# A fused retention, expert and MLP kernel: the MLP reads its tokens in the order in which the experts store them

## The reference

```python
# 1. retention: 4 batches x 8 heads x 768 steps, head dimension 64
state = gamma * state + outer(k[t], v[t]);  y[t] = (q[t] @ state) / 8
# 2. mixture of experts, one expert of 8 for each token (x: 3072 x 512)
e_idx  = argmax(x @ w_gate);  probs = softmax(x @ w_gate)
eom    = sigmoid(x @ w_output_gate)
out[t] = probs[t, e] * eom[t, e] * (relu(x[t] @ w1[e]) @ w2[e])   # 512 -> 1024 -> 512
# 3. gated MLP on all tokens
xn  = x / sqrt(mean(x * x) + 1e-6) * rms_g
g   = xn @ w_gate2;  out = (g * sigmoid(g) * (xn @ w_val)) @ w_out   # 512 -> 1536 -> 512
```

## Time and profile before

| | |
|---|---|
| the profiled execution's own time | 1163.04 us |
| its span, first to last instruction | 1161.2 us |
| mean granted TensorE clock | 0.989 |
| PE busy | 1119.0 us, 96% of the span |
| PEld busy | 936.0 us, 81% |
| DVE busy | 432.2 us, 37% |
| ACT busy | 384.2 us, 33% |
| POOL busy | 135.2 us, 12% |

### The profile page before, as it was taken

How to read it: one execution, slowest core, us unless ns; L and a number is a source line. 1 busy time by engine, 2 the same in 40 slices (tenths; PEclk the granted TensorE clock), 3 DMA queues, 4 the chain that set the end, 5 groups by cost and what they waited for, 6 DMA issues and landing times.

```text
span 1161.2 us, 19477 instructions
## 1 busy us (share of the span) xinstructions
PE 1119.0 (96%) x6051; PEld 936.0 (81%) x6052; DVE 432.2 (37%) x812; ACT 384.2 (33%) x632; POOL 135.2 (12%) x188
## 2 busy tenths in 40 slices
PE   6999998999999999994999999999999999999997
PEld 5999986888888888883888888888888888888886
DVE  3777753423415415312443323322332332233222
ACT  2554432534435435423324213212231322222112
POOL 2444423201001101101100100000010010000000
PEclk9999999999999999997999999999999999999999
DMA  9989814435333533532200200020020001000001
GB/s 195 250 238 243 218 56 154 142 95 178 108 108 121 186 108 118 190 94 70 79 31 1 74 1 1 2 71 0 0 72 0 0 19 53 0 0 37 1 1 37
DMA packets 111244, 97.22 MB, mean 84 GB/s; under 512 B 79968, under 2 KB 85344, under 8 KB 111200
## 3 DMA queue, kind: packets, MB, share of 16 engines
q1 hardware_dynamic: 98624, 67.12, 20.3%
q0 software_dynamic: 6528, 21.50, 6.0%
q10 hardware_dynamic: 6048, 8.01, 2.1%
HBM read 76.43 MB, written 20.19 MB: 83 GB/s over the span
## 4 chain that ended last, share of the span: by engine, by line
PE 51%; issue 2%; ACT 1%; DMA 1%; DVE 1%; POOL 0%; POOLq 0%; SPq 0%; ACTq 0%
PE bank L630 17%; PE bank L631 17%; PE bank L632 17%; PE bank L622 0%; DVE hl L1206 0%; ACT hh L884 0%; DMA yr<-expert_rows,cur_idx 0%; DMA out_rows<-x_out 0%; POOL yr L1349 0%; ACT x_out L891 0%; ACT junk L859 0%; DVE xl L1189 0%; ACT xh L869 0%; DVE yr L1184 0%; ACT small L862 0%
## 5 line engine op out<-in xcount | busy, mean ns | idle before, releaser
L1197 DVE TENSOR_TENSOR gated<-bank,sig 128x512 f32<-128x512 f32 x72 | 49.8, 691 | 311.7 <-ACT sig L877 311.7
L630 PE MATMUL bank<-xh,w1h 128*128 128x512 f32 x384 | 149.4, 389 | 0.0
L632 PE MATMUL bank<-xh,w1l 128*128 128x512 f32 x384 | 149.4, 389 | 0.0
L631 PE MATMUL bank<-xl,w1h 128*128 128x512 f32 x384 | 149.4, 389 | 0.0
L877 ACT ACTIVATE sig<-bank 128x512 f32<-128x512 f32 x72 | 43.1, 598 | 273.2 <-PE bank L632 273.0
L630 PE MATMUL bank<-w2h,hh 128*128 128x512 f32 x288 | 113.2, 393 | 4.4 <-DVE hl L1206 4.4
L631 PE MATMUL bank<-w2l,hh 128*128 128x512 f32 x288 | 112.1, 389 | 0.0
L632 PE MATMUL bank<-w2h,hl 128*128 128x512 f32 x288 | 112.1, 389 | 0.0
L1042 DVE TENSOR_TENSOR hidl<-bank,hidh 128x512 fp32r<-128x512 f32 x58 | 39.7, 685 | 162.0 <-ACT hidh L769 162.0
L884 ACT ACTIVATE hh<-prod 128x512 fp32r<-128x512 f32 x72 | 45.5, 632 | 153.5 <-PE bank L632 133.0
L1206 DVE TENSOR_TENSOR hl<-prod,hh 128x512 fp32r<-128x512 f32 x72 | 49.9, 693 | 95.0 <-ACT hh L884 95.0
(11 more groups left out here) (185 smaller groups left out, 1881.3 us busy)
## 6 DMA issues: line engine op xcount, KB each, us to landing
stage<-in_moe_w SPq DMA_DIRECT2D x64, 512.0 KB, 5.3
expert_rows<-tile_o ACTq DMA_DIRECT2D x29, 256.0 KB, 2.3
q_raw<-in_q SPq DMA_DIRECT2D x24, 256.0 KB, 5.6
k_raw<-in_k SPq DMA_DIRECT2D x24, 256.0 KB, 6.3
v_raw<-in_v SPq DMA_DIRECT2D x24, 256.0 KB, 3.8
out_rows<-x_out SPq DMA_DIRECT2D x24, 256.0 KB, 2.8
stage<-in_moe_w_out SPq DMA_DIRECT2D x6, 512.0 KB, 3.3
stage<-in_moe_w_gate SPq DMA_DIRECT2D x5, 512.0 KB, 6.7
```

What stands on the lines that cost most here:

```text
L630: pe.matmul(out_ap, lh, rh, start=first, stop=False)
L631: pe.matmul(out_ap, lh, rl, start=False, stop=False)
L632: return pe.matmul(out_ap, ll, rh, start=False, stop=last)
L1197: v3.tensor_tensor(gated[:], bank[GV[f % 2][0]][:, :], sig[:], ALU.mult).then_inc(s["gated_done"], 1)
```

## The change

1. **Layout.** `y_dram` has 3200 rows in all. Each tile is stored right behind the rows of the experts ahead of it, so that row i of y_dram is the i-th token in expert order. The tail of a tile that an expert doesn't fill is overwritten by the next store. The routing gets some ten instructions more for `row_at`, between `index_ready` and `control_ready`.
2. **Row data.** For every token its factor and its number are stored as two words at its place in expert order (`row_meta`), by 24 indexed stores of POOL, three behind each of eight row fetches. They are read back by one DMA of 3072 pieces of 8 bytes. `gates_of_rows` gets three instructions more for the places.
3. **Loads of a block.** Blocks 1 to 5 come by one plain DMA of 1 MB each from SP in place of four gathers of POOL.
4. **Block 0** is loaded ahead of the fetch for tile 19, into the buffers `x_out` and `more_rows`; its statistics and scaling stand ahead of tile 22, half of its transposes behind tile 22, the rest behind tile 23, in PSUM banks 6 and 7. Tiles 22 and 23 are written out behind the loop.
5. **Stores.** The MLP's rows leave by indexed stores of POOL, from four buffers in place of two.
6. **Beginning.** The zero rows are written from ACT's queue behind the constants; the constants are reordered and come in four DMAs.
7. **fetch_rows(3)** stands ahead of the wait for `gates_ready`.

```diff
+XG_AT = 54 * 1024
+ROWS_FROM = SURE - 5
+FINAL_AFTER = 13
...
-        y_dram = nc.dram_tensor("expert_rows", (EXPERTS * CAP, D), U32).ap()
+        y_dram = nc.dram_tensor("expert_rows", (TOKENS + P, D), U32).ap()
+        meta_dram = nc.dram_tensor("row_meta", (TOKENS, 2), U32).ap()
...
+        def turned_bank(n, kd):
+            return bank[6 + kd % 2] if isinstance(n, int) and n == 0 else bank[GV[kd // 2][kd % 2]]
... SP
-            for e in range(2):
-                sp.dma_start(x_dram[ds(e * CAP, 1), :], no_row).then_inc(s["bases_set"], 16)
...
-            def store_block(n):
-                for t in range(BLK):
-                    sp.wait_ge(s["sum_out"], BLK * n + t + 1)
-                    sp.dma_start(out[ds((n * BLK + t) * P, P), :], x_rows[:, t % 2, :]).then_inc(out_stored[t % 2], 16)
+            def load_rows(n):
+                sp.wait_ge(s["xn_turned"], KD * n)
+                sp.dma_start(yr[:].bitcast(U32), y_dram[ds(n * BLK * P, BLK * P), :].rearrange("(t p) d -> p t d", p=P))\
+                  .then_inc(s["yrows_in"], 16)
+            sp.wait_ge(s["tile_stored"], 16 * TILES)
+            with sp.Fori(1, NBLK) as n:
+                load_rows(n)
... PE
-            with pe.Fori(LEAD, SURE) as a:
+            with pe.Fori(LEAD, SURE - 2) as a:
                 expert_tile(a)
+            expert_tile(SURE - 2)
+            turn_xn(0, [0])
+            expert_tile(SURE - 1)
+            pe.wait_ge(s["xl_ready"], 2)
+            turn_xn(0, [1])
...
-                if f == 0 and not (isinstance(n, int) and n == 0):
+                if f == 0 and isinstance(n, int) and n == 0:
+                    pe.wait_ge(s["tile_stored"], 16 * TILES)
+                elif f == 0:
                     pe.wait_ge(s["sum_out"], BLK * n)
...
-            turn_xn(0, [0, 1])
             ffn_block(0)
... ACT
+            with act.Fori(LEAD, SURE - 2) as a:
                 expert_tile(a)
+            act.wait_ge(s["early_done"], 2)
+            norm_stats(0)
+            expert_tile(SURE - 2)
+            turned_hi(0, 0)
+            turned_hi(0, 1)
+            expert_tile(SURE - 1)
+            turned_hi(0, 2)
+            turned_hi(0, 3)
...
-                    if t >= 2 or not (isinstance(n, int) and n == 0):
-                        act.wait_ge(out_stored[t % 2], 16 * ((BLK // 2) * n + t // 2))
-                    nc.scalar.activation(x_rows[:, t % 2, :], bank[SUM[t]][:, :], ACT.Copy).then_inc(s["sum_out"], 1)
+                    if not (isinstance(n, int) and n == 0):
+                        act.wait_ge(out_stored[t], 16 * n)
+                    nc.scalar.activation(out_rows(t), bank[SUM[t]][:, :], ACT.Copy).then_inc(s["sum_out"], 1)
... DVE, between index_ready and control_ready
-            also(v3.tensor_copy(row_at[:, LEAD:], src_f[0:1, LEAD:]))
+            settle(v3.tensor_tensor_scan(upto_n[:], scan_ones[:], n_e[:], 0.0, ALU.mult, ALU.add))
+            settle(v3.tensor_tensor(ahead_e[:], upto_n[:], n_e[:], ALU.subtract))
+            also(...back_e...); also(memset); also(memset)
+            settle(v3.scalar_tensor_tensor(out=skip_e[:, 1:], ...), 4)
+            settle(v3.tensor_tensor(by_skip[:], begun[0:1, :, :], ..., ALU.mult))
+            settle(v3.tensor_reduce(skip_f[:], by_skip[:], X, ALU.max))
+            settle(v3.tensor_tensor(at_f[:], con[0:1, C_ROW:C_ROW + TILES + 1], skip_f[:], ALU.subtract))
+            settle(v3.tensor_scalar(row_at[:, LEAD:], at_f[:, LEAD:], lead_n[0:1, 0:1], None, ALU.add))
...
+            dve.wait_ge(s["meta_in"], 16)
+            settle(v3.tensor_copy(row_scale[:], meta_back[:, :, 0]))
+            stage_scale(0)
+            normalise(0)
+            expert_tile(SURE - 2)
+            turned_lo(0, 0)
+            turned_lo(0, 1)
+            expert_tile(SURE - 1)
+            turned_lo(0, 2)
+            turned_lo(0, 3)
... POOL
             pool.wait_ge(s["control_ready"], 1)
+            fetch_rows(LEAD + 1)
             pool.wait_ge(s["gates_ready"], 1)
             load_early(0)
-            fetch_rows(LEAD + 1)
+            fetch_rows(LEAD + 2)
...
+            for i in range(UNITS // 3):
+                fetch_rows(LEAD + 4 + i)
+                for u in range(3 * i, 3 * i + 3):
+                    scatter_meta(u)
+            with pool.Fori(LEAD + 4 + UNITS // 3, ROWS_FROM) as a:
+                fetch_rows(a)
+            pool.wait_ge(s["meta_stored"], 16 * UNITS)
+                pool.dma_start(meta_back[:].bitcast(U32), meta_dram.rearrange("(j p) c -> p j c", p=P))\
+                  .then_inc(s["meta_in"], 16)
+            pool.wait_ge(s["tile_stored"], 16 * FINAL_AFTER)
+            pool.wait_ge(s["early_done"], 2)
+            pool.dma_start(x_rows[:].bitcast(U32), y_dram[0:2 * P, :].rearrange("(t p) d -> p t d", p=P))\
+              .then_inc(s["rows0_in"], 16)
+            pool.dma_start(more_rows[:].bitcast(U32), y_dram[2 * P:4 * P, :].rearrange("(t p) d -> p t d", p=P))\
+              .then_inc(s["rows0_in"], 16)
+            pool.wait_ge(s["meta_in"], 16)
+            nc.gpsimd.tensor_copy(out_idx[:], meta_back[:, :, 1].bitcast(U32)).then_inc(s["ids_ready"], 1)
+            with pool.Fori(ROWS_FROM, SURE) as a:
                 fetch_rows(a)
...
+                    pool.wait_ge(s["sum_out"], BLK * n + t + 1)
                     pool.sem_inc(s["stood"], 1)
-                    nc.gpsimd.indirect_dma_start(yr[:, t, :].bitcast(U32), None, y_dram, ...)
+                    nc.gpsimd.indirect_dma_start(out, bass.IndirectOffsetOnAxis(cur_idx4[:, t:t + 1], 0),
+                                                 out_rows(t), None).then_inc(out_stored[t], 16)
```

More of the change, by code:

```diff
@@ L612, in _ @@
             tile_if_real(TILES - 1)
-            def turn_xn(n, halves):
-                for t in range(BLK):
-                    pe.wait_ge(s["norm_done"], BLK * n + t + 1)
-                    for half in halves:
-                        for i in range(2):
-                            kd = 2 * half + i
-                            mm = pe.transpose(bank[GV[half][i]][:, t * P:(t + 1) * P],
-                                              yr[:, t, kd * P:(kd + 1) * P], ident)
-                            if t == BLK - 1:
-                                mm.then_inc(s["xn_turned"], 1)
             def three(out_ap, lhs, rhs, first, last):
@@ L905, in ffn_block @@
                 sums_out(n)
-            act.wait_ge(s["rms_in"], 16)
-            act.wait_ge(s["rest_in"], 16)
-            nc.scalar.activation(table_in[:], con[:, C_EPS:C_EPS + 1], ACT.Sqrt).then_inc(s["stood"], 1)
-            norm_stats(0)
-            for kd in range(KD):
-                turned_hi(0, kd)
             ffn_block(0)
@@ L1128, in gates_of_rows @@
                 settle(v3.tensor_reduce(chosen[:], eg[:], X, ALU.add))
-                settle(v3.tensor_tensor(row_scale[:], chosen[:], gsum[:], ALU.mult))
+                also(v3.tensor_tensor(meta[:, :, 0], chosen[:], gsum[:], ALU.mult))
+                settle(v3.tensor_tensor(back[:], onehot[:], back_e[:, :].unsqueeze(1).to_broadcast([P, UNITS, EXPERTS]),
+                                        ALU.mult), 2)
+                settle(v3.tensor_reduce(back_f[:], back[:], X, ALU.add))
+                settle(v3.tensor_tensor(meta_idx[:], slot_f[:], back_f[:], ALU.add))
                 dve.sem_inc(s["gates_ready"], 1)
@@ L1149, in _, with stage_scale, normalise, turned_lo @@
             gates_of_rows()
-            with dve.Fori(LEAD, SURE) as a:
-                expert_tile(a)
+            def stage_scale(n):
+                if not (isinstance(n, int) and n == 0):
+                    dve.wait_ge(s["mult_ready"], BLK * n)
+                v3.tensor_copy(bscale[:], row_scale[:, ds(n * BLK, BLK)]).then_inc(s["scale_staged"], 1)
+            def normalise(n):
+                for t in range(BLK):
+                    one = slice(t, t + 1)
+                    dve.wait_ge(s["root_done"], BLK * n + t + 1)
+                    v3.reciprocal(inv[:, one], root[:, one]).then_inc(s["inv_done"], 1)
+                    dve.wait_ge(s["inv_done"], BLK * n + t + 1)
+                    v3.tensor_tensor(mult[:, one], inv[:, one], bscale[:, one], ALU.mult).then_inc(s["mult_ready"], 1)
+                    dve.wait_ge(s["mult_ready"], BLK * n + t + 1)
+                    rows = block_rows(n, t)
+                    v3.tensor_scalar(rows, rows, mult[:, one], None, ALU.mult)\
+                      .then_inc(s["norm_done"], 1)
+            def turned_lo(n, kd):
+                dve.wait_ge(s["xh_ready"], KD * n + kd + 1)
+                v3.scalar_tensor_tensor(out=xl[:, kd, :], in0=turned_bank(n, kd)[:, :], scalar=rms[:, kd:kd + 1],
+                                        in1=xh[:, kd, :].bitcast(F32), op0=ALU.mult, op1=ALU.subtract)\
+                  .then_inc(s["xl_ready"], 1)
+            with dve.Fori(LEAD, SURE - 2) as a:
+                expert_tile(a)
+            dve.wait_ge(s["meta_in"], 16)
[8 more added lines that the diff above has]
```

(1 more changed line is left out.)

251 lines of the change are left out of this document (136 added, 115 removed).

## The result

The changed kernel took 1156.64 us (median of 4 runs, 1155.16 to 1156.99); the kernel before took 1163.06 us beside it (4 runs, 1162.61 to 1164.81). The ratio is 0.994, with a 95% interval of 0.9922 to 0.9957. It is faster by 6.4 us. The profiled execution took 1156.39 us with a span of 1154.6 us, at a mean clock of 0.992.

A forecast was written before the change was run, and what follows sets the result against it. PE, busy 96% of the span, was taken as the bound. Pause -14.7, transposes +1.8, ACT +0.6, fetch -5.9, beginning -1.2, end +1.7 sum to -17.7 us: 1163.04 to 1145.3 us, range 1142.0 to 1151.0.

The forecast's parts named there:

- The end (part 5): End of the span: POOL's last indexed store lands later than the plain store did; 1.7 us lost, bounds 0.4 to 3.5.
- Statistics and copies on ACT: Tiles 22 and 23: block 0's statistics and copies make ACT late for relus; 0.6 us lost, bounds 0 to 1.5.
- the pause: Between last expert tile and block 0: 14.7 us gained, 6.4 us of PE pause stay, half-clock loss unchanged at 1.6 us.
- rival (a): Tile 19's row fetch a few microseconds late behind the read-back, PE waits 5 us; total near 1150 us; chance 0.13.
- So nothing is late next: After tile 3's earlier fetch: tile 4's fetch still arrives in time, so nothing of the gain is lost.
- What costs nothing: Block stores, 1 MB block loads and the 24 row data stores fit in idle time: 0, with 1 us allowed either way.
- The 5.9 us of the fetch: Tile 2 to tile 3: the earlier fetch removes a 4.34 us PE wait and 1.5 us of low clock; 5.9 us gained.
- The beginning: Start of kernel: q, k and later loads start earlier once zero-row stores leave SP's queue; 1.2 us gained, bounds 0 to 1.3.
- the read-back: Ahead of tile 19's fetch: 3072 pieces of 8 bytes take up to 8 us, within about 12 of room; cost 0.
- (c): Not faster: the read-back at 171 ns a piece takes 33 us and delays tile 19's rows; total 1165 us; chance 0.03.
- Rival (b): Pause lasts until POOL's start at 540.04 and ACT collisions reach their bounds, 2.9 and 0.9 us; total 1149.1; chance 0.12.
- Rival (d): Before block 0: the clock stays up over the shorter pause; total 1143.7 us; chance 0.07.

The follow-up runs named there:

- e1: Kernel before plus one small DMA of 2 KB issued by POOL after the last bank copy; 1168.99 us, single execution.
- e2: Kernel before plus a POOL copy of 128 words after the last bank copy, no DMA; 1171.95 us, single execution.
- e3: Changed kernel with the last block stored by SP as plain DMAs in token positions, placing of the last 512 rows left out; 1153.04 us, single execution.
- e4: Changed kernel with block 0's statistics ahead of tile 20, transposes behind tiles 20 and 21; 1154.88 us, single execution.
- e7: Kernel before with only the zero-row stores on ACT's queue and the fetch for tile 3 ahead of both waits; 1160.44 us, ratio 0.9955.
- e6: Changed kernel without the 24 row data stores and their read-back, so rows are scaled and placed wrongly; 1156.85 us, single execution.
- e0: Changed kernel unedited, timed again beside e9 on the same chip; 1159.02 us, ratio 0.9941 to the kernel before.
- e5: Changed kernel with the second load of MLP weights and POOL's split of it one tile later; 1159.58 us, ratio 0.9953 to the kernel before.
- e9: Changed kernel with e4's earlier preparation, e5's later split, and row data stores kept out of tiles 7 and 11; 1152.84 us, ratio 0.9891 to the kernel before.
- e8: Kernel before with e7's two edits, plus the second MLP weight load and split one tile later; 1159.62 us, ratio 0.9942.

## Why the prediction was wrong

**The step that failed most: "The end (part 5)", +1.7 us.** It took the landing of the last indexed store as the end of the span. The issues came as told (1.27 us apart), and the landing was faster than the row I took: 2.7 us at the median, not 3.83. The estimate by the Trainium skill ("DMA: Bandwidth & Descriptors", section "Anatomy of one DMA — SWDGE (gpsimd) path"), 2.6 us, agrees with the trace. But the span doesn't end when the data has landed. It ends when POOL's closing drain has, 6.8 us after its last operation, and that cost 4.7 us more than the term. No rival had it. The trace of before held it all the same: a drain of 10.6 us, hidden because POOL's work was over at 959. I asked where the stores land and not what POOL still does behind its last instruction. e1 and e2 show the cost in the kernel before, e3 shows it gone from the changed one.

**"Statistics and copies on ACT", +0.6 us, bounds 0 to 1.5.** The mechanism was the right one, the place too (tile 22, second relu, 1.44 us to spare). The size was 3.7 us: I counted the 5.5 us of the operations and neither the wait for DVE ahead of them, nor the issue behind, nor the clock that falls once PE waits 2.2 us. I had charged the clock for the pause and for rival (a), but not for this. e4, which moves the statistics off the tile with the weight pieces, takes the wait from 2.23 to 0.58 us, but adds 0.91 us in tile 23 and gives back only some 1.5 of the 3.7 us. So part of this cost is explained and part stays open. Why the 1.7 us of issue stands there was not tried.

**"So nothing is late next" and "What costs nothing", 0.** The 5.9 us of the fetch came in full. But the fetch that came earlier also pulled POOL's split onto DVE's, and so the last weight load of tile 3 went out 2.0 us late: 1.7 us back (2.1 in e7). I looked for the next fetch and not for the work that is queued behind it on POOL. The row stores were costed as POOL's time, and they are DMAs too: they delay the last weight piece of tiles 7 and 11 by 0.9 us each, and 1.8 us of waits there are gone in e6; that is over the 1 us that I allowed.

**What held.** The pause: 5.75 us where 6.4 were forecast, paced by PE's own count through the empty tiles, with the half clock at its end as in the kernel before. ACT came out of its tiles at 542.45, ahead of its first sigmoid, and there is no wait. The beginning: 1.24 us by the first products of tile 1. There the number held and my account of it didn't: PE's first operations came 2.28 us earlier, and 1.04 us of that were lost again with no new wait, since the next operations took longer: four transposes 1.06 us in place of 0.60. PE's first turning of unit 1, in the changed kernel and in the one before:

```profile
14.18 1.06 PE L438 MATMUL bank<-con,q_s 128*128 128x128 f32 x4
...
16.29 0.60 PE L413 MATMUL bank<-con,q_s 128*128 128x128 f32 x4
```

In both kernels the fast operations begin after 16.0 us. The profile's clock reads 1.00 there in both, so it doesn't name the cause. The transposes, the blocks and the read-back (9.2 us, no cost) were right as well. Rivals (a) and (c) fell: PE waits nowhere for the fetch of tile 19. (The price of (a) left out its own 1.5 us of clock; with it, it would have been near 1152, over the range.) Rival (b) had the right sign for its ACT part, at 0.9 us where 3.1 more came, and fell for the pause. Rival (d) fell: the clock did go down.

The errors share a direction. Of a sum of -17.7 us every term of gain was within 0.7 us, and what I charged for work on ACT, DVE and POOL was too small at every place: 4.7 us at the end, 3.1 at tile 22, 3.2 from tile 4 to 22.

## What to carry to other kernels

Before the last work of a kernel is moved to another engine, look at what that engine does between its last instruction and the end of the span; POOL needs some 7 us there, and with SP the end was 8.1 us shorter (e3), so the last stores belong to an engine with a short drain. When work is put into an idle stretch, measure the stretch from the last to the next operation with waits and issue counted, and put all of it where no weight load or split follows. When something on a queue comes earlier, list all that stands behind it on that queue, and see beside what it will now run.

## What the runs showed of the hardware that was not expected

- POOL's closing drain ends 6.8 us after POOL's last operation (1146.65 + 0.97 to 1154.4), 6.7 and 6.6 us after a small DMA (e1) and a copy of 128 words (e2), 7.7 us after a gather in the kernel before. ACT's took 0.6 us.
- A DVE operation of 1.22 us took 3.20 us beside one of POOL.
- ACT could begin with the last weight piece (512 KB) 3.5 to 3.8 us after its load was issued where neither POOL's MLP load nor the row stores stood beside it (before, e6, e7), 4.4 to 5.8 us beside the row stores (the change, e0, e5), and 4.3 to 5.0 us beside POOL's load of 512 KB (e5, e9, e8).
- Behind the wait of 2.2 us in tile 22 PE went to the half clock in all five profiles that have it (the tile took 17.1 to 17.2 us). Behind waits of 2.0 to 2.1 us in tile 4 it did so in e0 and e3 (16.1 us) and not in e4 and e7 (14.7 and 14.8).
- 3072 pieces of 8 bytes were read back in 9.2 us, where 171 ns a packet would have made 33.
- The kernel before had a median of 1163.1 us in the first comparison and of 1165.6 to 1166.0 on the three chips of the experiments; 3 us is half of a change of this size.
